# Weight sums made ahead of the second softmax, their high parts on ScalarE, and an earlier wait for one gate chunk

## The reference

```
qn = q / (norm(q, axis=1) + 1e-6);  kn = k / (norm(k, axis=1) + 1e-6)
s  = kn.transpose(0, 2, 1) @ qn / tau              # 256 x 256 per batch
a  = softmax(s, axis=-1)
x  = (v @ a).reshape(12032, 256)
x  = (sigmoid(x @ w_gate) * (x @ w_val)) @ w_out   # w_gate, w_val 256 x 1536
h  = x @ w_in                                      # w_in 256 x 2048
out = (h - tanh(h)) @ w2_out                       # w2_out 2048 x 256
```

## Time and profile before

| | |
|---|---|
| median of 3 runs | 2344.0 us (2343.25 to 2345.59) |
| the profiled execution | 2343.12 us, span 2341.3 us |
| TensorE busy | 2282.6 us, 97% |
| VectorE busy | 1373.5 us, 59% |
| ScalarE busy | 1089.0 us, 47% |
| GpSimd busy | 613.0 us, 26% |
| mean granted TensorE clock | 0.991 of full speed |

### The profile page before, as it was taken

How to read it: one execution, slowest core, us unless ns; L and a number is a source line. 1 busy time by engine, 2 the same in 40 slices (tenths; PEclk the granted TensorE clock), 3 DMA queues, 4 the chain that set the end, 5 groups by cost and what they waited for, 6 DMA issues and landing times.

```text
span 2341.3 us, 35799 instructions
## 1 busy us (share of the span) xinstructions
PE 2282.6 (97%) x12060; PEld 1979.0 (85%) x12060; DVE 1373.5 (59%) x2767; ACT 1089.0 (47%) x1956; POOL 613.0 (26%) x512
## 2 busy tenths in 40 slices
PE   8984999999999999999999999999999999999998
PEld 7874888888888888888998888888888888888898
DVE  6743565565565664655755656646556556556565
ACT  5533354454453453543544534535435445345354
POOL 3555131230230321311351303203113123022032
PEclk9996999999999999999999999999999999999999
DMA  9725232322331422323243314224232232232143
GB/s 340 210 75 196 83 102 75 111 94 65 119 102 50 134 74 78 110 78 97 96 134 104 102 49 134 87 65 131 66 89 99 76 112 94 64 120 93 48 135 102
DMA packets 240406, 245.58 MB, mean 105 GB/s; under 512 B 203360, under 2 KB 203616, under 8 KB 240352
## 3 DMA queue, kind: packets, MB, share of 16 engines
q1 hardware_dynamic: 235152, 225.39, 31.1%
q0 software_dynamic: 4400, 19.40, 2.4%
q10 hardware_dynamic: 800, 0.10, 0.0%
HBM read 225.18 MB, written 19.66 MB: 105 GB/s over the span
## 4 chain that ended last, share of the span: by engine, by line
PE 92%; DVE 2%; POOL 2%; DMA 2%; ACT 1%; issue 0%; SPq 0%; ACTq 0%; DVEq 0%; POOLq 0%
PE up L1105 53%; PE x_acc L1105 28%; PE acc L1105 10%; PE x_acc L1131 2%; DMA qk_in<-in_k 1%; DVE g_lo L911 1%; ACT func_out L641 1%; DVE up L907 1%; ACT g_hi L649 1%; POOL g L538 0%; POOL g L527 0%; DMA w_sums<-g 0%; POOL g L534 0%; POOL g L520 0%; POOL t_sums L530 0%
## 5 line engine op out<-in xcount | busy, mean ns | idle before, releaser
L555 POOL TENSOR_TENSOR g<-t_sums,g 128x512 fp32r<-128x512 f32 (+1 forms) x384 | 486.4, 1272 | 1602.9 <-ACT g L676 1602.9
L641 ACT ACTIVATE func_out<-up 128x512 f32<-128x512 f32 (+1 forms) x672 | 395.5, 589 | 708.0 <-PE up L1105 667.4
L907 DVE TENSOR_TENSOR up<-up,func_out 128x512 f32<-128x512 f32 (+1 forms) x288 | 197.6, 686 | 408.6 <-ACT func_out L641 407.5
L1105 PE MATMUL up<-x_lo,in_w_hi 128*128 128x512 f32 (+1 forms) x768 | 299.3, 390 | 38.3 <-DVE g L954 37.4
L1105 PE MATMUL x_acc<-g,w_ring 128*128 128x256 f32 (+1 forms) x2304 | 306.2, 283 | 0.0
L911 DVE TENSOR_TENSOR g_lo<-up,g_hi 128x512 fp32r<-128x512 f32 (+1 forms) x288 | 195.9, 680 | 179.5 <-ACT g_hi L649 179.3
L1105 PE MATMUL up<-x_hi,in_w_lo 128*128 128x512 f32 (+1 forms) x768 | 298.3, 388 | 0.0
L1105 PE MATMUL up<-x_hi,in_w_hi 128*128 128x512 f32 (+1 forms) x768 | 296.5, 386 | 0.0
L1105 PEld LDWEIGHTS x_acc<-g,w_ring 128*128 128x128 f32 x2304 | 288.9, 192 | 0.0
L676 ACT ACTIVATE g<-t_sums 128x512 fp32r<-128x512 f32 (+1 forms) x384 | 238.0, 620 | 108.3 <-DVE t_sums L958 107.8
L649 ACT ACTIVATE g_hi<-up 128x512 fp32r<-128x512 f32 (+1 forms) x288 | 169.5, 588 | 221.0 <-DVE up L907 220.8
(11 more groups left out here) (172 smaller groups left out, 3223.2 us busy)
## 6 DMA issues: line engine op xcount, KB each, us to landing
w_ring<-w_sums SPq DMA_DIRECT2D x192, 896.0 KB, 4.5
v_in<-in_v SPq DMA_DIRECT2D x176, 64.0 KB, 2.2
out_rows<-out_sb SPq DMA_DIRECT2D x176, 64.0 KB, 1.8
qk_in<-in_q SPq DMA_DIRECT2D x29, 384.0 KB, 4.2
qk_in<-in_k SPq DMA_DIRECT2D x29, 384.0 KB, 6.2
w_sums<-g POOLq DMA_DIRECT2D x4, 1792.0 KB, 6.9
w_stage<-in_moe_w_out POOLq DMA_DIRECT2D x4, 512.0 KB, 5.5
w_stage<-in_moe_w_gate POOLq DMA_DIRECT2D x3, 512.0 KB, 7.3
```

What stands on the lines that cost most here:

```text
L555: pool.tensor_tensor(lo[:, cut, 0:half], t_sums[:, first - T1:first - T1 + 2, 0:half], hi[:, cut, 0:half].bitcast(F32), ALU.subtract).then ...
L641: act.activation(func_out[:, half, cut], func_bank(kind, i, tile)[:, cut], ACT.Sigmoid if kind == "U" else ACT.Tanh).then_inc(func_made, 1)
L907: dve.tensor_tensor(bank_cut, bank_cut, func[:, cut], ALU.mult).then_inc(prod_made, 1)
L1105: mm = pe.matmul(psum, a, b, start=start and n == 0, stop=stop and n == 2, skip_group_check=shared_bank)
```

## The change

Three things. First, `combine_piece` is split in three: `sum_piece` (GpSimd, the four sums), `hi_of_comb` (ScalarE, the high parts, three Copies) and `lo_of_piece` (GpSimd, the low parts, the store and the next load). GpSimd makes the sums of two pieces, then the low parts of the two. `sum_piece` waits for the Gram matrices instead of the softmax; even pieces put their sums into a part of `qk_in` that later is x2_lo, odd ones into `t_sums`. ScalarE does its part after the high parts of chunks 5, 6, 9 and 10 of tile 0. Second, each piece has a store semaphore of its own, and every reader waits only for the piece it needs. Third, `after_u` also holds for chunk 13 of long tiles and for chunks 5 to 11 of the others.

```diff
+        COMB_AFTER = [5, 6, 9, 10]
...
             def load_first_w2(t, first=False):
                 if first:
                     sp.wait_ge(att_made, B * KC)
-                    for slot in range(PAIR_SLOTS):
-                        sp.wait_ge(comb_stored[slot], 16 * (COMBS // PAIR_SLOTS))
+                    sp.wait_ge(comb_stored[0], 16)
...
-            def load_rest_of_w2(t):
+            def load_rest_of_w2(t, first=False):
                 for m in range(PAIR_SLOTS, PAIRS):
+                    if first and m % 2 == 0:
+                        sp.wait_ge(comb_stored[m // 2], 16)
...
+            def sum_piece(q):
+                pool.wait_ge(w_loaded[(WHOLE + q) % 2], 16 * ((WHOLE + q) // 2 + 1))
+                if q == 0:
+                    pool.wait_ge(gram_made, B * CHUNKS)
+                    pool.wait_ge(sq_made, 2 * B * CHUNKS)
+                if q >= 2:
+                    pool.wait_ge(w_split, WHOLE + q - 1)
...
+                pool.tensor_tensor(s1, a21, a22, ALU.add).then_inc(comb_step, 1)
+                pool.tensor_tensor(s3, a11, a21, ALU.subtract).then_inc(comb_step, 1)
+                pool.wait_ge(comb_step, 3 * q + 1)
+                pool.tensor_tensor(s2, s1, a11, ALU.subtract).then_inc(comb_step, 1)
+                pool.wait_ge(comb_step, 3 * q + 3)
+                pool.tensor_tensor(s4, a12, s2, ALU.subtract).then_inc(comb_summed, 1)
+
+            def lo_of_piece(q):
...
+                pool.wait_ge(comb_hi_made, 3 * (q + 1))
+                pool.tensor_tensor(lo[:, :, A11], a11, hi[:, :, A11].bitcast(F32), ALU.subtract)
                 for r in range(2):
+                    pool.tensor_tensor(lo[:, r, A12:A22 + 1], a12_a22[:, r],
+                                       hi[:, r, A12:A22 + 1].bitcast(F32), ALU.subtract)
+                    last = pool.tensor_tensor(lo[:, r, S1:S4 + 1], sums_of[:, r],
+                                              hi[:, r, S1:S4 + 1].bitcast(F32), ALU.subtract)
+                last.then_inc(w_split, 1)
                 pool.wait_ge(w_split, n + 1)
                 pool.dma_start(w2_sums[2 * q:2 * q + 2].rearrange("r p f -> p r f"),
...
+                               ).then_inc(comb_stored[q], 16)
                 load_next(n)
...
+            for q in range(0, COMBS, 2):
+                sum_piece(q)
+                sum_piece(q + 1)
+                lo_of_piece(q)
+                lo_of_piece(q + 1)
...
(hi_of_pair, ScalarE)
-                elif not first:
+                elif first:
+                    act.wait_ge(comb_stored[COMBS - PAIR_SLOTS + m], 16)
+                else:
...
+            def hi_of_comb(q):
+                if q >= PAIR_SLOTS:
+                    act.wait_ge(comb_stored[q - PAIR_SLOTS], 16)
+                act.wait_ge(comb_summed, q + 1)
+                a11, a12_a22 = comb_rows(q)
+                hi = comb_out(q, HI)
+                act.activation(hi[:, :, A11], a11, ACT.Copy).then_inc(comb_hi_made, 1)
+                act.activation(hi[:, :, A12:A22 + 1], a12_a22, ACT.Copy).then_inc(comb_hi_made, 1)
+                act.activation(hi[:, :, S1:S4 + 1], comb_sums(q), ACT.Copy).then_inc(comb_hi_made, 1)
...
                     hi_of(t, j, tile)
+                    if first and j in COMB_AFTER:
+                        hi_of_comb(COMB_AFTER.index(j))
...
+                if first:
+                    act.wait_ge(w_split, WHOLE + COMBS - 1)
                 split_x2(t, tile)
...
-                if first:
-                    for slot in range(PAIR_SLOTS):
-                        act.wait_ge(comb_stored[slot], 16 * (COMBS // PAIR_SLOTS))
...
(sums_and_lo_of_pair, VectorE)
-                if not first_pair:
+                if first_pair:
+                    dve.wait_ge(w_split, PIECES)
+                else:
...
(U, TensorE)
-                        after_u = LEAD + 2 <= j <= J1 and tile in LONG
+                        after_u = LEAD + 2 <= j < (J1 + 2 if tile in LONG else J1)
```

More of the change, by code:

```diff
@@ L212, in attn_two_mlp_kernel, with comb_rows, comb_lower, comb_sums @@
         HI, LO = 0, 1
+        def comb_rows(q):
+            rows = w_stage[(WHOLE + q) % 2].rearrange("p (r a f) -> p r a f", r=2, a=2)
+            return rows[:, :, 0, 0:P], rows[:, :, 1, :].rearrange("p r (o c) -> p r o c", o=2)
+        def comb_lower(q):
+            rows = w_stage[(WHOLE + q) % 2].rearrange("p (r a f) -> p r a f", r=2, a=2)
+            return rows[:, :, 0, P:2 * P]
+        def comb_sums(q):
+            flat = (t_sums[:, :, :].rearrange("p t c -> p (t c)") if q % 2 else
+                    qk_in[:, :, :, :, :].rearrange("p b w n c -> p (b w n c)")[:, 5120:6144])
+            return flat.rearrange("p (r o c) -> p r o c", r=2, o=4)
+        def comb_out(q, part):
+            return g2[:, q % PAIR_SLOTS, :].rearrange("p (r a o c) -> p r a o c", r=2, a=2,
+                                                      o=PRODUCTS)[:, :, part]
         first_sum = kept
@@ L264, in attn_two_mlp_kernel @@
         t_sums_made, t_hi_made, t_lo_made = sem("t_sums_made"), sem("t_hi_made"), sem("t_lo_made")
-        comb_step = sem("comb_step")
-        comb_stored = [sem(f"comb_stored{n}") for n in range(PAIR_SLOTS)]
+        comb_step, comb_summed, comb_hi_made = (sem("comb_step"), sem("comb_summed"),
+                                                sem("comb_hi_made"))
+        comb_stored = [sem(f"comb_stored{n}") for n in range(PAIRS // 2)]
         ring_loaded = [sem(f"ring_loaded{n}") for n in range(PAIR_SLOTS)]
@@ L432, in load_then_store @@
                     load_first_w2(t, first)
-                load_rest_of_w2(t)
+                load_rest_of_w2(t, first)
                 store(t, b_store, store_tile)
@@ L499, in split_piece @@
                 load_next(n)
[L501 to L532, removed]
-                for r in range(2):
[L534 to L540, removed]
@@ new lines, in sum_piece @@
+            def sum_piece(q):
[6 more added lines that the diff above has]
+                a11, a12_a22 = comb_rows(q)
+                a12, a22 = a12_a22[:, :, 0], a12_a22[:, :, 1]
+                a21 = comb_lower(q)
+                s1, s2, s3, s4 = (comb_sums(q)[:, :, o] for o in range(4))
+                pool.tensor_tensor(s1, a21, a22, ALU.add).then_inc(comb_step, 1)
[4 more added lines that the diff above has]
+                pool.tensor_tensor(s4, a12, s2, ALU.subtract).then_inc(comb_summed, 1)
@@ new lines, in lo_of_piece @@
+            def lo_of_piece(q):
+                n = WHOLE + q
+                a11, a12_a22 = comb_rows(q)
+                hi, lo, sums_of = comb_out(q, HI), comb_out(q, LO), comb_sums(q)
+                pool.wait_ge(comb_hi_made, 3 * (q + 1))
+                pool.tensor_tensor(lo[:, :, A11], a11, hi[:, :, A11].bitcast(F32), ALU.subtract)
+                for r in range(2):
+                    pool.tensor_tensor(lo[:, r, A12:A22 + 1], a12_a22[:, r],
[3 more added lines that the diff above has]
+                last.then_inc(w_split, 1)
@@ L544, in combine_piece @@
                                                                   ).bitcast(F32)
-                               ).then_inc(comb_stored[q % PAIR_SLOTS], 16)
+                               ).then_inc(comb_stored[q], 16)
                 load_next(n)
@@ L563, in _ @@
                 split_piece(n)
-            for n in range(WHOLE, PIECES):
-                combine_piece(n)
+            for q in range(0, COMBS, 2):
[3 more added lines that the diff above has]
+                lo_of_piece(q + 1)
             with pool.Fori(0, TILES_BATCH - 1) as t:
```

## The result

| | before | changed |
|---|---|---|
| median of 4 runs each | 2344.7 us (2343.3 to 2345.6) | 2305.2 us (2303.7 to 2305.5) |
| profiled execution's span | 2341.3 us | 2301.9 us |
| mean granted TensorE clock | 0.991 | 0.998 |

The ratio is 0.9831 (95% interval 0.9814 to 0.9848): 1.7% faster, 39.5 us by the medians. The forecast was 2304 (2298 to 2311).

The account below looks back on a forecast made before the run. TensorE, busy 97%, can save time only where idle or at its lower clock, chiefly a 40.0 us hole in tile 0. 2343.1 - 35.45 - 4.4 = 2303.3, predicted as 2304 against the median of 2344.0; range 2298 to 2311.

Parts of the forecast that it names:

- part 1: Tile 0: weight sums made at once remove the 40.0 us hole but add a 4.55 us stall, -35.45 us.
- the new stall: Tile 0: TensorE waits 4.55 us at D(11) because piece 3's sums delay ScalarE's sigmoid of chunk 11; bounds 1.0 and 6.5.
- (c): Tile 0: stall 6.5 us or a store as late, plus 2.4 at half clock; 2308.4, up to 2312; chance 0.16.
- The read port: Tile 0: two-input VectorE passes and GpSimd exclude each other; GpSimd's sums 0.5 to 2 us later, left in the range.
- part 2: Long tiles: chunk 13's gate half waits for the product only; 0.22 us in each of 20, 4.4 us, bounds 0 and 9.0.
- P3's wait: Long tiles: P3 waits for VectorE's low part of P1 (301.94), so 0.22 of the 0.45 us is kept.
- the hole of 40.0 us: TensorE in tile 0 before O(0): 37.6 us of idling plus 2.4 us at half pitch.
- the last stores: Tile 0: stores of pieces 2 and 3 done at 171.4 and 177.1, each 0.7 us before ScalarE asks.
- (b): Long tiles: the whole 0.45 us per tile is kept; 2299.4; chance 0.09.
- (a): Tile 0: loads do not suffer from the stores, stall 1.0 us instead of 4.55; 2300.5; chance 0.14.
- (d): Long tiles: the earlier start of chunk 13 gives nothing, P3 or another wait takes all; 2308.4; chance 0.08.
- (e): Tile 0: GpSimd stretches beside busy VectorE and TensorE until slower than before; 2353 at 3 times; chance 0.02.

Follow-up runs that it names:

- e1: The changed kernel with chunk 13 waiting for the low part of chunk 12 again, so the weight sums alone: 2312.6 us, ratio 0.9865.
- e2: The kernel before with only the TensorE part of the change, the earlier start of chunk 13: 2337.5 us, ratio 0.9973.
- e5: The changed kernel with ScalarE's high parts of pieces 0 and 1 one chunk earlier (after chunks 4, 5, 9, 10): 2297.2 us, ratio 0.9799.
- e3: The changed kernel with GpSimd issuing each next load ahead of the store of sums instead of behind it: 2306.5 us, ratio 0.9838.
- e9: The changed kernel itself, unaltered, run again beside two variants on one chip: 2305.8 us, ratio 0.9837.
- e4: The changed kernel with GpSimd's low parts of piece 1 waiting until VectorE has finished the second batch's logits: 2308.0 us, ratio 0.9848.
- e8: The changed kernel with loads ahead of stores and GpSimd's low parts of piece 3 after VectorE's vt passes: 2301.3 us, ratio 0.9818.
- e6: The changed kernel with loads ahead of stores, low parts of piece 1 after VectorE's logits, of piece 3 after its vt passes: 2305.4 us, ratio 0.9837.
- e7: The changed kernel with high parts after chunks 4, 5, 9, 10, loads ahead of stores, piece 3's low parts after vt passes: 2298.1 us, ratio 0.9807.

## Why the prediction was right, point by point

**Sum: right for partly wrong reasons.** The sums were forecast to give 35.45 us and gave 32.0 (e1); the earlier wait 4.4 and gave 7.1 (e2). The sum of 39.85 meets the measured 39.5 only because one error offsets the other.

**The walk through tile 0** held in its structure:

| | predicted | measured |
|---|---|---|
| high parts of piece 0 ready | 136.2 | 136.4 |
| load of piece 2 issued, landed | 141.95, 150.05 | 142.14, 150.3 |
| load of piece 3 issued, landed | 148.5, 156.6 | 148.60, 158.4 |
| sigmoid of chunk 10 | 154.7 | 155.92 |
| sums of piece 3 ready | 159.5 | 161.4 |
| sigmoid of chunk 11 | 161.2 | 163.29 |
| D(11) | 164.06 | 166.01 |

One wait was not where it was forecast. ScalarE did not wait for the sums of piece 2, which were done at 153.33. It was late itself, since its first exponential of the second softmax had waited 3.87 us, to 149.39, for VectorE's slow logits passes, and it began the high parts at 154.14; so the sigmoid of chunk 10 is 1.2 us later than forecast. The wait for the sums of piece 3 came as forecast (3.63 us, to 161.50).

**The mis-sized term in part 1 is the new stall**, 4.55 us forecast, 6.5 measured (166.01 - 159.50, of which 0.2 is the later start of the span). The load of piece 3 took 9.8 us, not 8.1: my value came from loads with nothing but a store ahead, and here the v transfers ran beside it as well. Whether they make the difference stays open: in e5 the load of piece 2 took 9.2 us behind its store with none beside it. The prediction's bound for loads of 10 us had just this stall of 6.5. e3 shows that ahead of the store the load lands in 4.7.

**The clock** was left out of the likeliest case and put into rival (c); it fell. Nine spacings at the lower level, 1.2 GHz, take 3.75 us instead of 9 x 0.227 = 2.04, so it cost 1.7. 40.0 - 6.5 - 1.7 = 31.8, against 32.0 in e1. That the two meet so closely is partly chance: the half clock lasts longer in some executions, and by the same working it cost 2.4 us in the traced one of e1 and 2.6 in that of e9. Behind the old hole it had cost 2.4. The rows before had shown the clock still up 4.8 us into the idle time and my stall was given as equally long; that was the moment to put the fall into the sum, at even odds, not at 0.16.

**The read port was looked at from the wrong side.** I weighed how far VectorE slows GpSimd (0.5 to 2 us; in fact GpSimd's low parts of pieces 0 and 1 took 4.6 us, as beside an idle VectorE, those of piece 2 5.0). It was VectorE that was blocked: two passes of 0.5 us each took 5.2 together (e4 undoes it). The runs show that GpSimd's instructions are the cause; that the two share a port is no reading of a trace. The Trainium skill's rule ("SBUF — State Buffer", "Who interferes with whom") names both directions; e3 (4.77 us), e4 (0.99 for the two passes) and e8 (0.68) agree with it. In the changed kernel this stop is hidden by the one at D(11), so it did not enter the sum.

**The mis-sized term in part 2 is P3's wait.** Mechanism and place were right, 0.22 us per tile was not: 0.36 alone (e2) and 0.40 in the changed kernel (tiles 91.11 apart, 91.51 before). I had read the release of P3 off tile 1, the first of the loop, where VectorE's low part of P1 ended 3.94 us after ScalarE's start on P1 (298.00 to 301.94). In tile 2 of the same trace it is 3.77 (389.49 to 393.26), as in all that I looked at later:

```profile
389.49 0.60 ACT L641 ACTIVATE func_out<-up 128x512 f32<-128x512 f32 x1 [0.19 <-PE up L1105]
```

```profile
392.58 0.68 DVE L965 TENSOR_TENSOR g<-up,g 128x512 fp32r<-128x512 f32 x1
```

With 3.77 the same working gives 0.39. Why tile 1 is slower by 0.17 us there stays open. Being the first of the loop is not enough: tile 1 is slower in the kernel before and in e2, but not in the changed kernel (265.81 to 269.58, 3.77) nor in e1, which has the new weight sums with the old wait.

**Right without reserve:** the hole of 40.0 us, that the early buffers allow it, no wait on the last stores, nothing gained in the tiles with short chunks (90.51 us before and after), and the stop at chunk 13 gone. Of the rivals, (c) came true in its stall of 6.5 us and in its clock, (b) nearly in its size, and they offset each other; (a), (d) and (e) did not happen. A granted clock below 1.00 in tile 0 stood among the prediction's signs of being wrong, and it came; the stop at P3, 0.06 us, is shorter than the 0.1 to 0.25 that it gave as a sign of being right.

## What to carry to other kernels

When work moves to an engine that runs in order, walk every instruction of the chain with its start, and put the new wait before the latest moment at which it costs nothing: here one chunk earlier (e5, ratio 0.9799) was worth more than the swapped load and both waits together (e6, 0.9837), and their intervals are apart. Before swapping two transfers in a queue, ask who waits for the one that is put off. Read a per-tile term off several tiles, not off one. And when GpSimd's work is moved out of a hole, look at which VectorE passes with two SBUF inputs it will run beside.

## What of the hardware was not expected

- VectorE can be starved through a whole string of GpSimd instructions, not just one: a pass of 0.68 us took 4.77 beside five of GpSimd's low parts (e3), two of 0.5 took 5.2 to 5.5 (changed kernel, e3), while GpSimd's took 0.74 and 1.29 as ever.
- A 512 KB load took 4.6 to 5.6 us with its store behind it (e3, e6, e7, e8) and 8.1 to 9.9 with the store in front (changed kernel, e1, e4, e5).
- The length of a stop alone did not decide whether the granted clock fell: behind a stop of 2.5 us at chunk 10 it fell in e8 and stayed up in e3, and behind waits of 4.5 and 4.3 us at D(11) the lower level lasted 3.5 us in the changed kernel and over 5 in e9, which is the same kernel.
